# A recurrent attention and two expert layers on one core: visits at other slots, and two operands copied by ScalarE in place of second loads

## The reference

```
for t in range(S):
    cur = einsum('bhd,bhe->bhde', u[None] * kt, vt)
    y[:, :, t] = einsum('bhd,bhde->bhe', rt, state + cur)
    state = wt[:, :, :, None] * state + einsum('bhd,bhe->bhde', kt, vt)
x = y, transposed to (3072 tokens, 384)
h = x @ w_in;  g = max(h, 0) + alpha * min(h, 0);  x = g @ w_out      # 384 -> 2048 -> 384
h = x @ w_in2; g = h * clip(h + 3, 0, 6) / 6;      out = g @ w_out2   # the same sizes
```

## Time and profile before

| | |
|---|---|
| three runs | 961.89, 963.04, 963.94 us, median 963.04 |
| the profiled execution | 963.65 us, its span 961.7 us |
| PE busy | 938.2 us, 98% of the span |
| DVE, ACT, POOL busy | 590.8 (61%), 317.0 (33%), 50.4 (5%) us |
| chain that ended last | PE 84%, DVE 2%, issue 1%, ACT 1% |
| granted clock of PE | 0.81 on the mean of the first 45 us, then 1.00 |
| loads and stores | 59.75 MB, mean 62 GB/s |

### The profile page before, as it was taken

How to read it: one execution, slowest core, us unless ns; L and a number is a source line. 1 busy time by engine, 2 the same in 40 slices (tenths; PEclk the granted TensorE clock), 3 DMA queues, 4 the chain that set the end, 5 groups by cost and what they waited for, 6 DMA issues and landing times.

```text
span 961.7 us, 23774 instructions
## 1 busy us (share of the span) xinstructions
PE 938.2 (98%) x10708; PEld 784.9 (82%) x10708; DVE 590.8 (61%) x894; ACT 317.0 (33%) x628; POOL 50.4 (5%) x38
## 2 busy tenths in 40 slices
PE   6979999999999999999999999999999999999998
PEld 5879888888888888888888888888888888888886
DVE  6776958755775686397448994544445445445443
ACT  4655453334253534423433321222122212112211
POOL 0000000000000000000006860000000000000000
PEclk7999999999999999999999999999999999999999
DMA  6952071043005202500005330010010100000000
GB/s 177 273 163 75 4 210 51 3 140 88 35 22 153 88 3 67 161 35 2 3 1 197 99 132 1 1 66 0 1 66 1 35 32 0 33 1 1 33 1 33
DMA packets 18740, 59.75 MB, mean 62 GB/s; under 512 B 2416, under 2 KB 2672, under 8 KB 18640
## 3 DMA queue, kind: packets, MB, share of 16 engines
q1 hardware_dynamic: 18640, 58.25, 20.4%
HBM read 48.80 MB, written 9.44 MB: 61 GB/s over the span
## 4 chain that ended last, share of the span: by engine, by line
PE 84%; DVE 2%; issue 1%; ACT 1%; DVEq 0%
PE banks L1041 38%; PE banks L1026 37%; PE banks L904 4%; PE banks L972 1%; PE banks L956 1%; PE banks L917 1%; PE banks L984 1%; PE banks L931 1%; DVE S L702 0%; DVE S L704 0%; DVE pos L768 0%; DVE A L666 0%; ACT Yt L488 0%; ACT pos L529 0%; DVE gh L772 0%
## 5 line engine op out<-in xcount | busy, mean ns | idle before, releaser
L1041 PE MATMUL banks<-gh,wsp 128*128 128x512 f32 (+1 forms) x1248 | 397.7, 376 | 0.9 <-DVE y2T L810 0.9
L1041 PEld LDWEIGHTS banks<-gh,wsp 128*128 128x128 f32 x1248 | 230.3, 188 | 44.5 <-issue 1.8
L1041 PE MATMUL banks<-gl,wsp 128*128 128x512 f32 (+1 forms) x624 | 232.8, 373 | 1.0 <-issue 1.0
L784 DVE SCALAR_TENSOR_TENSOR pos<-pos,banks 128x512 f32<-128x512 f32 x96 | 66.0, 688 | 175.2 <-ACT pos L538 175.2
L538 ACT ACTIVATE pos<-banks,three 128x512 f32<-128x512 f32 x96 | 66.2, 690 | 284.0 <-PE banks L1026 284.0
L1026 PE MATMUL banks<-xh_even,wsp 128*128 128x512 f32 (+1 forms) x672 | 153.7, 364 | 0.4 <-ACT xh_even L494 0.3
L768 DVE SCALAR_TENSOR_TENSOR pos<-neg,minus_slopes,pos 128x512 f32<-128x512 f32 (+1 forms) x112 | 86.2, 770 | 109.2 <-ACT pos L529 108.7
L1026 PE MATMUL banks<-xh_odd,wsp 128*128 128x512 f32 x576 | 148.5, 393 | 0.1
L1041 PEld LDWEIGHTS banks<-gl,wsp 128*128 128x128 f32 x624 | 117.6, 188 | 19.6
L1026 PEld LDWEIGHTS banks<-xh_even,wsp 128*128 128x128 f32 x672 | 114.0, 188 | 20.5 <-ACT xh_even L494 0.9
L1026 PEld LDWEIGHTS banks<-xh_odd,wsp 128*128 128x128 f32 x576 | 106.8, 188 | 22.7 <-issue 0.6
(11 more groups left out here) (71 smaller groups left out, 650.7 us busy)
## 6 DMA issues: line engine op xcount, KB each, us to landing
stage<-in_w_dram SPq DMA_DIRECT2D x32, 384.0 KB, 5.2
K<-in_k_dram SPq DMA_DIRECT2D x12, 448.0 KB, 3.8
W<-in_w_dram SPq DMA_DIRECT2D x12, 448.0 KB, 4.4
R<-in_r_dram SPq DMA_DIRECT2D x12, 448.0 KB, 7.6
KU<-in_k_dram SPq DMA_DIRECT2D x11, 448.0 KB, 4.3
A<-in_r_dram SPq DMA_DIRECT2D x11, 448.0 KB, 6.3
V<-in_v_dram SPq DMA_DIRECT2D x12, 384.0 KB, 7.4
xin<-x_dram SPq DMA_DIRECT2D x6, 768.0 KB, 5.9
```

The source lines that it names most:

```text
L784: nc.vector.scalar_tensor_tensor(out=pos[:, j], in0=pos[:, j], scalar=6.0, in1=psum[i % HR], op0=ALU.min, op1=ALU.mult).then_inc(g_ready, 1)
L1041: last = nc.tensor.matmul(psum[YBANK + window][:, 0:n], w_[a][:, window * 128:(window + 1) * 128], g_[b], start=(f == 0 and j == 0), stop= ...
```

## The change

Three things change. The slots: in unit 0 the last five visits move by one slot; from step 1 on the later visits of a step get other distances. The tiles of make_ku and make_ru change in units 0 and 1. And from step 1 on KU and RU are not loaded: ACT copies the plain tokens from K and R, and multiplies the others from K and R. Step 0 keeps its loads. DVE's first in-place multiplications of K and R now wait until KU and RU are ready.

```diff
-    AT_FIRST = (0, 4, 7, 10, 13, 14, 15, 16, 18, 20)
-    AT_SECOND = (-8, -6, 0, 4, 8, 11, 13, 14, 15, 16, 19, 21, 22, 24, 25)
-    AT_STEP = (-5, -4, 0, 5, 7, 10, 12, 14, 15, 16, 18, 19, 21, 23, 25)
+    AT_FIRST = (0, 4, 7, 10, 13, 15, 16, 17, 19, 21)
+    AT_SECOND = (-8, -6, 0, 4, 8, 11, 13, 14, 15, 16, 18, 20, 22, 23, 25)
+    AT_STEP = (-5, -4, 0, 5, 7, 10, 12, 14, 15, 16, 18, 20, 22, 23, 25)
...
-    U_AT = {N: (9, 8, 12) if N == 0 else (11, 11, 13) for N in range(NC - 1)}
+    U_AT = {N: ((10, 8, 12), (9, 12, 13))[N] if N < 2 else (11, 11, 13) for N in range(NC - 1)}
...
-                for f, load_it in zip(range(8, 14), (load_ku, load_ru, load_k, load_w, load_r, load_v)):
+                for f, load_it in zip(range(8, 12), (load_k, load_r, load_w, load_v)):
                     next_tile(f)
                     load_it(1, 0)
-                for f in range(14, NT):
+                for f in range(12, NT):
                     next_tile(f)
                 load_k(1, 1)
-                load_ku(1, 1)
                 load_w(1, 1)
-                load_ru(1, 1)
...
+                def plain(x, to, par, gs):
+                    nc.scalar.copy(of_parity(to, par, gs), of_parity(x, par, gs))
...
                 def make_ku(c, gs):
-                    of_streams(act, loaded_ku, c, gs)
-                    times_u(KU, 1, c, gs).then_inc(ku_ready, 1)
+                    if c:
+                        for g in gs:
+                            act.wait_ge(kv_filled, 2 * (c - 1) + g + 1)
+                        of_streams(act, loaded_k, c, gs)
+                        plain(K, KU, 0, gs)
+                        times_u(K, KU, 1, gs).then_inc(ku_ready, 1)
...
                 def make_ru(c, g):
-                    of_streams(act, loaded_ru, c, (g,))
-                    times_u(RU, 0, c, (g,)).then_inc(ru_ready, 1)
+                    if c:
+                        act.wait_ge(ya_filled, 2 * (c - 1) + g + 1)
+                        of_streams(act, loaded_r, c, (g,))
+                        plain(R, RU, 1, (g,))
+                        times_u(R, RU, 0, (g,)).then_inc(ru_ready, 1)
...
                         of_streams(dve, loaded_w, c, gs)
+                        if c:
+                            dve.wait_ge(ku_ready, c + 1)
...
                         of_streams(dve, loaded_r, c, gs)
+                        if c:
+                            dve.wait_ge(ru_ready, 2 * c + g)
```

More of the change, by code:

```diff
@@ L271, in load_k @@
                     load(K[0:PP], rows_of(k, c, g), c, g, loaded_k)
[L273 to L281, removed]
                 def load_r(c, g):
@@ L316, in _ @@
                 next_tile(2)
-                load_ku(0, 1)
-                load_ru(0, 1)
+                load(KU[0:PP], rows_of(k, 0, 1), 0, 1, loaded_ku)
+                load(RU[0:PP], rows_of(r, 0, 1), 0, 1, loaded_ru)
                 sp.wait_ge(scored, scored_at(0, 4, 0))
@@ L345, in _ @@
                         for g in BOTH:
-                            load_ku(c, g)
                             load_w(c, g)
                         for g in BOTH:
-                            load_ru(c, g)
                             load_v(c, g)
@@ L398, in of_pair, with of_parity, times_u @@
                     return x.rearrange("p (b q) i -> p b q i", q=NQ)[:, :, q]
-                def times_u(x, par, c, gs):
-                    x = columns(x, gs).rearrange("p (q i e) -> p q i e", i=TB, e=2)[:, :, :, par]
+                def of_parity(x, par, gs):
+                    return columns(x, gs).rearrange("p (q i e) -> p q i e", i=TB, e=2)[:, :, :, par]
+                def plain(x, to, par, gs):
+                    nc.scalar.copy(of_parity(to, par, gs), of_parity(x, par, gs))
+                def times_u(x, to, par, gs):
                     for q in range(NQ):
-                        last = nc.scalar.mul(of_pair(x, q), of_pair(x, q), u_col[0:PP, q:q + 1])
+                        last = nc.scalar.mul(of_pair(of_parity(to, par, gs), q), of_pair(of_parity(x, par, gs), q), u_col[0:PP, q:q + 1])
                     return last
                 def make_ku(c, gs):
-                    of_streams(act, loaded_ku, c, gs)
-                    times_u(KU, 1, c, gs).then_inc(ku_ready, 1)
-                def make_ru(c, g):
-                    of_streams(act, loaded_ru, c, (g,))
-                    times_u(RU, 0, c, (g,)).then_inc(ru_ready, 1)
+                    if c:
[4 more added lines that the diff above has]
+                        times_u(K, KU, 1, gs).then_inc(ku_ready, 1)
+                    else:
+                        act.wait_ge(loaded_ku[1], 16)
+                        times_u(KU, KU, 1, gs).then_inc(ku_ready, 1)
+                def make_ru(c, g):
+                    if c:
[3 more added lines that the diff above has]
+                        times_u(R, RU, 0, (g,)).then_inc(ru_ready, 1)
+                    else:
+                        act.wait_ge(loaded_ru[1], 16)
+                        times_u(RU, RU, 0, (g,)).then_inc(ru_ready, 1)
                 def split_hi(f):
```

## The result

The changed kernel takes 967.02 us (median of 10 runs, 964.34 to 969.47), the kernel before 962.63 us (10 runs, 961.89 to 965.43). The ratio is 1.0043, 95% interval 1.0030 to 1.0056: slower by 4.4 us, by more than the 0.2% that can be told. The profiled execution has a span of 965.3 us. A run takes a little longer than its span: 1.9 us in the kernel before and 2.3 us in the changed one, the same within 0.1 in every run whose span is on record. So 0.4 of the 4.4 us lie outside the span, where no row shows them, and 4.0 us inside.

The account below looks back on a forecast made before the run. PE, busy throughout the steady unit, bounds the kernel, with no slack from t1 through ACT and DVE to the next unit's first hidden burst. 4.4 - 0.7 - 2.3 + 0.5 + 0.6 = +2.5 us gives 965.5 us, range 961.8 to 968.2.

Parts of the forecast that it names:

- Part 1: Units 2 to 4: two ACT copies ahead of tile 14's activation delay xl and PE one to one, +4.4 us.
- rival 4: Units 2 to 4: ACT's copies are covered by slack, 961.1 us, or 957.7 with early gains; chance 0.15.
- Part 2: Units 2 to 4: y0 one burst later no longer waits for the state, -0.7 us.
- Part 3: Unit 0: fewer loads end instruction stalls at level 4 (1.75) and partly in a result burst (0.55), -2.3 us.
- Part 4: Rest of unit 0: the 1024-column copy eats y's earlier start, a 512-column copy delays the end, +0.5 us.
- Part 5: Unit 1: y0 waits for DVE's state, +1.2, partly offset by shorter t0 and t1 waits; +0.6 us.
- Rival 2: Unit 0's instruction stalls stay, perhaps from another cause, so the loads term is 0: 967.8 us; chance 0.17.
- Rival 3: Units 0 and 1: shorter waits reach the unit ends, -1.5 and -0.8, so 962.1 us, no change; chance 0.23.

Follow-up runs that it names:

- run 3: Changed kernel without its copies of the plain tokens into KU and RU, so its diagonal scores of steps 1 to 5 are not the reference's: 961.18 us.
- run 2: Changed kernel with the old slots and old tiles of make_ku and make_ru, so only the loads are replaced by copies: 970.35 us.
- run 4: Changed kernel with, in units 2 to 4, make_ku at tile 9 and make_ru at tiles 12 and 13, all copies still made: 962.71 us.
- run 1: Kernel before with the new slots and new tiles of make_ku and make_ru alone; KU and RU still loaded, nothing copied: 964.67 us.
- run 9: Kernel before once more, no edit, for its profile alone: single time 963.26 us.
- run 10: Changed kernel once more, no edit, for its profile alone: single time 967.43 us.
- run 7: Kernel before without the 20 loads of KU and RU, nothing in their place, K and R in the later order; not the reference's scores: 959.97 us.
- run 5: Changed kernel with the step 1 loads behind tiles 10 to 13, order K, W, R, V, in place of 8 to 11: 965.54 us.
- run 6: Changed kernel with later K and R loads, and make_ku at tile 9, make_ru at 12 and 13 for units 1 to 4: 959.45 us.
- run 8: Changed kernel with late K and R loads, products at tiles 9, 12, 13, and step 1's slots as in the kernel before: 958.47 us.

## Why the prediction was right, and where it was not

The forecast was slower by 2.5 us, 965.5 us; it is slower by 4.4 us. The direction and its main cause held, and one term failed. That the time still fell into the range is in part luck: units 1 to 4 gave 0.5 us less than forecast, which took back some of the miss.

**Part 1 held.** 4.4 us forecast, in units 2 to 4; 4.7 us by run 3, 4.5 by run 2. The row of 1007 ns for 1024 columns was a good neighbour of the 1.12 us measured. The waits for xh and xl are where they were looked for, at tile 13, 1.3 us each, and run 4 shows that nothing but the place ahead of tile 14's activation made the copies cost: rival 4, that they are covered, was wrong for this place and right for tile 9. DVE's new waits cost nothing (runs 1 and 3), and nor did the second copy of 512: without all the copies a unit gains 1.56 us, and the two ahead of xh are 1.57.

**Part 2 held.** -0.7 us forecast, -1.0 by run 1, with the earlier trace rows gone.

**Part 3 failed, and is nearly all of the miss.** The step reads "The first, 1.7 us, stays, because K and R now come where KU and A came; and DVE's full 20.4 us would hide its loss." The -2.3 was the sum of 1.75 us at level 4 and 0.55 in the result burst, with nothing for level 1. Three things in it were off. First, the 2.75 us of late stalls were one execution's: 0.24 and 0.77 us stood there in the other two profiles of the kernel before, so 1.3 on the mean of the three. Second, the level 1 stall did not simply stay. The place of the two loads in the queue is the same, their time is not: K and R are issued 6 us earlier (runs 9 and 10). The stall was 2.85 and 1.97 us in the two profiles after and 1.6 to 2.1 in runs 2 to 4, which have these early loads too; with the old loads it was 1.70, 1.21, 1.16 and, in run 1, 2.19. The means are 2.1 and 1.6 us, but the single values overlap, so that the early loads made it longer is likely and not shown. Third, DVE did not hide it: in the stretch of the first row it is busy for 16.44 us and not 20.32. The stalls at level 0, 1.19 and 0.94 us in the two profiles after, are not the early loads' alone: run 7, with late loads, has 0.47 us there, and runs 2 to 4, with early ones, have none of 0.2 us or more.

What the runs show in place of -2.3: +0.8 us from the first hidden burst to level 4 over nine profiles, in which the stall of the result burst lies, and at level 4 a stall of 0.9 us (mean of three) less, so about 0. By the medians, parts 3 and 4 together gave +0.2 us for a forecast of -1.8, 2.0 too little. Units 1 to 4 gave 3.8 for 4.3, and 0.4 us lie outside the span; 2.5 + 2.0 - 0.5 + 0.4 is 4.4. The mechanism, instruction fetches that queue behind loads, was right (the packets above, runs 5 and 7), and with the order of run 7 the saving is 2.8 us. The change does not have this order.

Rival 2, the stalls stay, was forecast at 967.8 and is nearest to the time. Its reason, another cause than the loads, is refuted by run 5 and the packets. Part 3 says that the sum with 0 for it would end at +4.7; its terms give +4.8, and with them the 967.8 of rival 2. Rival 3, that the early gains carry to the ends of units 0 and 1, did not come about: unit 1 is 0.2 us longer and not 0.8 shorter.

The Trainium skill, "Runtime: NRT & Kernel Launch", section "Instruction fetch mechanics", has each engine fetch its instructions in 16 KiB blocks over a DMA queue of its own, with the boundary's cost mostly hidden. The trace agrees with the size: 84 packets with 1.38 MB, 16.4 KB each. It is hidden in the steady units, where PE has no wait for its own instructions from 200 to 500 us; while loads fill the engines, PE loses 1.2 to 2.9 us at level 1.

**Part 4 held.** From level 4 to the end of unit 0, without the stall at level 4, it was 32.3, 32.3 and 32.7 us in the three profiles before and 33.0 and 32.9 in the two after: +0.5 us, as forecast. Of its halves the slots gave -0.5 us (run 1, 31.9 us without its stall) to -1.0 (run 3, 31.4 us), and the copies took +1.5 (run 3 against the changed kernel). PE's wait for y2T grew from 0.63 us to 1.3, so visits that come earlier end in a longer wait there.

**Part 5: the right cause at the wrong visit.** I looked for y0 waiting over 1 us for the state. PE's waits in unit 1 are

```profile
PE banks L940 <- DVE S L713: 0.8, 1, 0.8
...
PE banks L1050 <- DVE y2T L819: 0.6, 1, 0.6
PE banks L965 <- DVE xl_odd L719: 0.5, 1, 0.5
```

L940 is kv1: moved one burst earlier, it waits itself for DVE to read the bank of the visit ahead, so y0 behind it is no longer early. The waits for Yt are gone, y1 waits 0.5 us in place of the 0.3 forecast. The unit grew by 0.2 us on the means, where 0.6 was forecast, less than it varies.

**What stays open.** Why the clock falls behind the level 1 stall. Of nine profiles with a stall of 1.1 us or more there, eight show it (all but the first of the kernel before, with 1.70 us); of four without the stall, none. In run 2 the clock fell behind a wait of another kind too, 1.70 us for Yt, and in run 1 it did not behind 1.6 us of the same wait; so the fall needs no instruction stall, and such a stall does not always bring it. No run varied the stall alone. Open too are the 0.4 us outside the span (runs 1 and 7, edits of the kernel before, are like it in this; runs 2 to 6 and 8 are like the changed kernel, run 3 without copies too), and how much the early loads of K and R by themselves add at level 1.

## What to carry to other kernels

Work that is taken from an idle engine or queue and given to another costs what it delays on that engine, so look first for what stands behind it in program order; here 1.5 us of copies on an engine busy a third of the time cost 1.5 us a unit ahead of the hand-over to the next unit, and nothing with one part two tiles earlier and the rest behind the hand-over. When a load is removed, ask when the ones that take its place in the queue are issued, by what they wait for, and not only where they stand: here one wait of 5.0 us had held back all behind it. And a term that rests on a stall in one profile wants a second profile first: the 2.75 us of late stalls were 0.24 and 0.77 us in the next two.

## What the runs showed of the hardware

PE's instructions come in packets of 16 KB, one for about 255 of its instructions, on a DMA queue of their own, and the packets queue with the loads. With loads ahead (DMA share 1.04 in the kernel before) the packet for the level 1 visit began 4.5 to 6.2 us after PE had started the 126 matmuls before, and PE stood still for 1.2 to 2.9 us; the stall ended 1.3 to 1.6 us after the packet. The stalls sit at the same matmuls in every execution and change in length (1.70, 1.21, 1.16 us at level 1 in the kernel before). Issuing two loads of 448 KB 15 and 21 us later takes the one at level 1 away (run 5).

Behind such a stall the granted clock of PE fell to its lower level (1.2 GHz) for 3.4 us in eight of nine profiles, though PE was busy again by then: in the profile after, a result burst took 1.92 us there and 1.08 us where the clock held. If the fall belongs to the stall, the stall costs more than its own length.
